# Attention, Fourier and MLP kernel on one core: xs·at behind ak·va on TensorE, y behind m2's copy on VectorE, xs2 without its wait for y

## The reference

```python
B, H, S, D = 4, 8, 768, 40
for t in range(S):
    y[:, :, t] = einsum('bhd,bhde->bhe', rt, state)
    Sa = einsum('bhde,bhe->bhd', state, at)
    state_decay = state * wt[:, :, None, :] - einsum('bhd,bhe->bhde', Sa, bt)
    state = state_decay + einsum('bhd,bhe->bhde', vt, kt)
# then: x = y as (B, S, 320); u = x + real(fft(fft(x, axis=1), axis=2));
# x = u + relu(norm(u) @ w_ch1) @ w_ch2; then a token MLP and a channel MLP
```

## The kernel before

| block | row in the profile | what it is | who reads it |
|---|---|---|---|
| m2 | ps<-mt,nn | step of the inverse | DVE mt<-ps,mt (L432) |
| rhs_v | pr<-va,ak | ak times va, 16 products of 64x40, fp32 | rhs_a adds to the same bank |
| n8 | ps<-nn,nt | last squaring, bf16 | DVE nn<-ps,eye (L436), "n8's copy" |
| rhs_a | pr<-xs,at | at times xs, added to rhs_v's bank | ACT rhs_b (L341) |
| ut | ps<-ident_a,u (L711) | 4 transposes of u | ACT ut (L356) |
| tokk | ps<-ident_a,kt (L719) | 4 transposes of kt | ACT tok_of |
| m3 | pp<-mt,nn | last product of the inverse | ACT minv (L335) |
| abk | pp<-at,bt and pp<-at,kt | first block of the next window | DVE aa, ak |

## Time and profile before

### The profile page before, as it was taken

How to read it: one execution, slowest core, us unless ns; L and a number is a source line. 1 busy time by engine, 2 the same in 40 slices (tenths; PEclk the granted TensorE clock), 3 DMA queues, 4 the chain that set the end, 5 groups by cost and what they waited for, 6 DMA issues and landing times. The chain is left out here.

```text
span 1011.8 us, 48583 instructions
## 1 busy us (share of the span) xinstructions
PE 958.3 (95%) x21467; PEld 911.6 (90%) x21468; DVE 500.4 (49%) x941; ACT 349.0 (34%) x758; POOL 301.7 (30%) x361
## 2 busy tenths in 40 slices
PE   6899999999999679998999999999999999999995
PEld 4788988888888568888999999999999999999995
DVE  4366677766767356765444333346733223322330
ACT  3466666665665433332221111232322112211220
POOL 6456655565566417705200000027500000000000
PEclk9999999999999999999999999999999999999998
DMA  7256666676665344302000000003100000000000
GB/s 250 101 185 210 196 198 202 196 229 209 199 211 174 96 122 156 102 1 68 25 0 0 0 0 0 0 0 107 37 1 20 20 0 19 19 19 6 13 19 19
DMA packets 50249, 86.80 MB, mean 86 GB/s; under 512 B 6066, under 2 KB 29746, under 8 KB 50194
## 3 DMA queue, kind: packets, MB, share of 16 engines
q1 hardware_dynamic: 48578, 81.96, 25.5%
q0 software_dynamic: 880, 3.69, 1.2%
q10 hardware_dynamic: 736, 0.48, 0.2%
HBM read 70.37 MB, written 7.86 MB: 77 GB/s over the span
## 5 line engine op out<-in xcount | busy, mean ns | idle before, releaser
L1412 ACT ACTIVATE d_h_hi<-d_bank 128x384 fp32r<-128x384 f32 x96 | 47.1, 491 | 200.1 <-PE d_bank L1494 200.1
L1449 DVE SCALAR_TENSOR_TENSOR d_h_lo<-d_bank,d_h_hi 128x384 fp32r<-128x384 f32 x96 | 53.5, 558 | 78.1 <-ACT d_h_hi L1412 78.1
L1508 PE MATMUL d_bank<-w_lo,d_h_hi 128*128 128x320 f32 x288 | 89.0, 309 | 0.0
L1508 PE MATMUL d_bank<-w_hi,d_h_lo 128*128 128x320 f32 x288 | 89.0, 309 | 0.0
L1508 PE MATMUL d_bank<-w_hi,d_h_hi 128*128 128x320 f32 x288 | 89.0, 309 | 0.0
L1412 ACT ACTIVATE c_h_hi<-c_bank 128x384 fp32r<-128x384 f32 x80 | 37.5, 489 | 146.4 <-PE c_bank L1494 146.4
L1508 PE MATMUL c_bank<-w_hi,c_h_hi 128*128 128x320 f32 x240 | 74.8, 312 | 0.0
L1508 PE MATMUL c_bank<-w_hi,c_h_lo 128*128 128x320 f32 x240 | 74.1, 309 | 0.0
L1508 PE MATMUL c_bank<-w_lo,c_h_hi 128*128 128x320 f32 x240 | 74.1, 309 | 0.0
L1461 DVE TENSOR_TENSOR d_o<-d_bank,u_all 128x320 f32<-128x320 f32 x24 | 11.8, 492 | 111.0 <-PE d_bank L1508 111.0
L1449 DVE SCALAR_TENSOR_TENSOR c_h_lo<-c_bank,c_h_hi 128x384 fp32r<-128x384 f32 x80 | 42.3, 554 | 40.9 <-ACT c_h_hi L1412 40.9
(11 more groups left out here) (265 smaller groups left out, 2792.1 us busy)
## 6 DMA issues: line engine op xcount, KB each, us to landing
e_raw<-in_e SPq DMA_DIRECT2D x72, 256.0 KB, 4.3
r_raw<-in_c SPq DMA_DIRECT2D x24, 768.0 KB, 4.3
tok<-tok_of SPq DMA_DIRECT2D x24, 320.0 KB, 2.7
e_raw<-in_e SPq DMA_DIRECT2D x24, 260.5 KB, 4.1
va<-in_c SPq DMA_DIRECT2D x24, 160.0 KB, 2.5
vb<-in_c SPq DMA_DIRECT2D x24, 160.0 KB, 2.7
attention_out<-yout SPq DMA_DIRECT2D x92, 40.0 KB, 2.0
stage<-in_moe_w_ch POOLq DMA_DIRECT2D x4, 640.0 KB, 6.9
```

The costliest lines, as they stand in the source:

```text
L1412: nc.scalar.activation(h_hi[:, m, :], bank[m % 4][:, 0:TW], ACT.Relu).then_inc(h_hi_done, 1)
L1449: nc.vector.scalar_tensor_tensor(h_lo[:, m, :], bank[m % 4][:, 0:TW], 0.0, h_hi[:, m, :].bitcast(F32), ALU.max, ALU.subtract).then_inc(h_l ...
L1508: last = nc.tensor.matmul(bank[4 + t % 2][:, 0:E], lhs, rhs, start=(m == 0 and i == 0), stop=(m == NM - 1 and i == 2))
```

## The change

Three things change, all in the tables. In ORDER_PE, rhs_a stands directly behind rhs_v and n8 behind it. In ORDER_DVE, y stands behind m2 (m2's copy) instead of ahead of it. In PORT_AFTER, the entry of xs2 is gone. No instruction is added or removed, and the code of the blocks stays the same but for its place in the file.

```diff
-ORDER_DVE = [... ("u", -3), ("xs", -2), ("y", -4), ("m2", -2), ("n8", -2), ("suff", 0), ("aa", -1),
+ORDER_DVE = [... ("u", -3), ("xs", -2), ("m2", -2), ("y", -4), ("n8", -2), ("suff", 0), ("aa", -1),
...
-            ... ("xsd", -2), ("m2", -1), ("rhs_v", -1), ("n8", -1),
-            ("rhs_a", -1), ("ut", -2), ("tokk", 0), ("m3", -1)]
+            ... ("xsd", -2), ("m2", -1), ("rhs_v", -1), ("rhs_a", -1),
+            ("n8", -1), ("ut", -2), ("tokk", 0), ("m3", -1)]
...
-PORT_AFTER = {"kt": ("suff", 0), "mt0": ("decay", 1), "xs2": ("y", -2)}
+PORT_AFTER = {"kt": ("suff", 0), "mt0": ("decay", 1)}
```

More of the change, by code:

```diff
@@ L30 @@
 ORDER_SP = [("store", -5), ("cp", -4), ("vb", -4), ("va", -2), ("e", 0), ("rr", -3)]
-ORDER_DVE = [("du2", -3), ("m1", -2), ("xt", -4), ("u", -3), ("xs", -2), ("y", -4), ("m2", -2), ("n8", -2), ("suff", 0), ("aa", -1),
+ORDER_DVE = [("du2", -3), ("m1", -2), ("xt", -4), ("u", -3), ("xs", -2), ("m2", -2), ("y", -4), ("n8", -2), ("suff", 0), ("aa", -1),
              ("ak", -1), ("rv", -3), ("decay", 0), ("ru", -3)]
@@ L35 @@
             ("res2", -2), ("y_s", -3), ("n2", -1), ("y_k", -3), ("sol2", -2), ("n2t", -1), ("y_b", -3), ("m1", -1), ("res3", -2),
[2 rows of a table removed]
+            ("n4", -1), ("upd_k", -3), ("upd_b", -3), ("n4t", -1), ("sol3", -2), ("xsd", -2), ("m2", -1), ("rhs_v", -1), ("rhs_a", -1),
+            ("n8", -1), ("ut", -2), ("tokk", 0), ("m3", -1)]
 ORDER_ACT = [("rhs", -1), ("m3", -1), ("ut", -2), ("du0", -1), ("tokd", 0), ("tokb", 0), ("res1", -1), ("tokk", 0), ("du1", -1),
@@ L690, in unit @@
                 last.then_inc(ready["rhs_v"], 1)
[L691 to L697, removed]
             if name == "rhs_a":
@@ L705, in unit @@
                 last.then_inc(filled["rhs_a"], 1)
+            if name == "n8":
+                take(n, "xsd", -1)
+                for j, par in halves:
+                    q = tok_half(par)
+                    last = mm(out[q, j * C:j * C + C], nt[2][q, j, :], nn[2][q, j, :])
+                    took(n, 2 * j + par, last, ("xsd", -1))
+                last.then_inc(filled["n8"], 1)
             if name == "ut":
```

## The result

| | before | after |
|---|---|---|
| median | 1015.12 us (4 runs, 1013.65 to 1015.89) | 1030.87 us (4 runs, 1028.68 to 1033.6) |
| ratio | | 1.0158, 95% interval 1.0129 to 1.0187 |
| the profiled execution, its time / span | 1013.78 / 1011.8 us | 1028.68 / 1026.7 us |

The changed kernel is slower, as forecast. The forecast was 1028.9 us with a range up to 1031.0; the median of these runs is 1030.87 us, and the ratio on the base of the prediction, 1015.53 us, gives 1031.6 us, so the loss was 16.0 us (13.1 to 19.0) where 13.4 us had been worked out. The two profiled executions are 14.9 us apart.

The account below looks back on a forecast made before the run. TensorE's in-order list was taken to bound the attention; 12.2 us from tokk's waits, 0.6 us in the second window and 0.58 us behind the loop gave 13.4 us on the 1015.53 us median: 1028.9 us, range 1020.5 to 1031 us.

Parts of the forecast that it names:

- rhs_a waits for rhs_v's end (313.48 and not 313.11): On TensorE, rhs_a would start no earlier after the swap, so n8 leaves a free place for one paid for.
- tokk 0.58 us later, through n8's copy: At the window's end, n8 shifts 0.86 us, less 0.28 us its copy had waited; tokk loads at 315.27, not 314.69.
- The whole of it reaches abk: tokk's full 0.58 us delays abk's products through m3; the 0.50 us from m3 to abk is TensorE's own step.
- Part 2: y behind m2's copy on VectorE: costs nothing, worth only the 0.28 us already taken off tokk's delay.
- the 0.28 us taken off: Time n8's copy had waited on VectorE for m2's copy, subtracted from n8's shift of 0.86 us.
- Part 3: xs2 without its wait on GpSimd: earlier start buys nothing; xs ends at 313.10 instead of 312.98, covered.
- The cover I named, rhs_a's 0.27 us: Slack left between xs's end at 313.10 on VectorE and rhs_a's need of it at 313.37.
- The smaller and the larger loss: Rivals: rhs_a starts at 313.11 or at sets abk (17%); xs late for rhs_a, 1031 to 1033 us (6%).
- The sum, 13.4 us: Total attention loss: tokk's wait 21 times at 0.58 us (12.2 us), second window 0.6, window behind the loop 0.58.
- the first window's term: Loop's first window: loss 0, at most 0.6 us, since TensorE stands 1.54 us inside ut while n8's copy ends.
- the 0.5 us for the median: Allowance for the median within the forecast's own range of 1026.5 to 1030.5 us.
- The case 'faster', 3.7 us: Rival: n8's copy stops being late on VectorE and tokk's 0.16 us wait goes, 23 times; 1011.8 us, 5%.

Follow-up runs that it names:

- n8_twice: The changed kernel with n8's 16 products run once more between rhs_v and rhs_a; window 13.82 us, median 1030.63 us, ratio 1.0159.
- own_bank: The changed kernel with n8's products in another PSUM bank, so m3 and not tokk waits for n8's copy; window 13.32 us, median 1016.14 us.
- swap_only: The kernel before with only TensorE's order changed, rhs_a ahead of n8; window 13.80 us, median 1025.45 us, ratio 1.0111.
- no_swap: The kernel before with y behind m2's copy and xs2 without its wait, TensorE's order kept; window 13.39 us, median 1019.89 us, ratio 1.0058.
- y_early: The kernel before with y ahead of xt on VectorE and xs2 without its wait; window 13.20 us, median 1012.30 us, ratio 0.9972.

## Why the prediction was right or wrong

**rhs_a waits for rhs_v's end (313.48 and not 313.11): right**, shown by n8_twice and by the idle time of 0.27 us. The prediction called the 0.11 us of the earlier trace rows "again" the same step as the 0.15 us of the earlier trace rows; inside the loop it is 0.15 us in the changed kernel too (312.71 to 312.86).

**tokk 0.58 us later, through n8's copy: right.** It is 0.59 us by the two timelines, and own_bank takes 0.47 us out of the window when tokk does not wait.

**The whole of it reaches abk: right.** abk moved by 0.58 us, the window from 13.22 to 13.79 us.

**Part 2 costs nothing: right. That it is worth the 0.28 us taken off: wrong.** swap_only leaves y ahead of m2's copy and has the same window (13.80 against 13.79 us), with VectorE idle for 0.49 us ahead of n8's copy. n8 comes so late through the swap that its copy is clear of m2's copy wherever y stands. The 0.28 us belong to the swap, and the sum stays the same.

**Part 3, xs2's start buys nothing and is covered: right, with a wrong size.** xs got longer by 0.18 us, not 0.12, since it starts 0.42 us into xs2 and still ends 0.35 us behind it. For this reason m2's copy came only 0.22 us earlier against rhs_v, where 0.3 to 0.4 us were forecast. The Trainium skill, "SBUF — State Buffer", "Who interferes with whom", calls the shared port pair an exclusive lock over which such a pair of instructions contends; its words "for the whole instruction" stand there for the 2-port modes. Taken for the whole of xs, as the prediction took them, xs would have ended 0.49 us behind xs2; the rows show 0.34 or 0.35 us in each kernel, so what is excluded is less than the instruction. The cover I named, rhs_a's 0.27 us, was not the only place to look: n8's copy, the third instruction behind xs on VectorE, had no cover at all in the old order, as no_swap shows.

**The smaller and the larger loss:** neither came by its mechanism. Measured on the median the time lies where the larger loss was priced (1031 to 1033 us), but xs was never late for rhs_a. In the equal windows the granted clock stayed at 1.00 (77.53 to 312.02 us); low clock stood in the loop's first window (0.54 from 34 to 41 us in the first profile of the changed kernel, 1.00 in that of the kernel before) and behind the loop.

**The sum, 13.4 us: right for the equal windows, and close for the attention in part by luck.** The last y moved by 13.7 us on the mean of three profiles each. In the first profiles rhs_v number 2, 3 and 23 starts its products at 48.10, 61.53 and 325.85 us before, and at 49.91, 63.73 and 339.61 us after; the last y starts at 369.11 and 383.67 us. By stretches, the loss is:

| stretch | forecast, us | the profiled pair, us | mean of three, us |
|---|---|---|---|
| to the second rhs_v (the loop's first window) | 0, at most 0.6 | 1.8 | 0.6 |
| to the third rhs_v | 0.6 | 0.4 | 0.4 |
| the next 20 windows | 11.6 | 11.6 | 11.6 |
| from the 23rd rhs_v to the last y | 1.2 | 0.8 | 1.1 |
| together | 13.4 | 14.6 | 13.7 |
| from the last y to the end | 0 | 0.3 | -0.4 |

**The step that failed is what stands outside the equal windows: the first window's term, put at 0 (at most 0.6 us), and the 0.5 us for the median.** In the profiled pair the first term measured 1.8 us, with the clock as just said; in the three pairs of profiles it is 1.8, 0.8 and -0.8 us. The second term was too small: the profiled pair is 14.9 us apart and the medians 15.75 us, and the ratio on the base of the prediction makes it 16.0 us. The changed kernel's profiled execution (1028.68 us) was the fastest of its four, and the others, of which there is no trace, took 1029.84, 1031.89 and 1033.6 us at mean granted clocks of 0.984, 0.980 and 0.977, against 0.985. Where their time went is not known.

Twelve runs of the kernel before went from 1010.72 to 1018.6 us in one series, and the medians of the changed kernel in two series were 1030.87 and 1025.83 us. The first ratio, 1.0158, says 16.0 us and the second, 1.0135, says 13.7 us; the intervals overlap, and 13.4 us lies in both. So it is in part chance that the time came out above the range and not in it. With 2 to 3 us for the spread, and not 0.5, the upper end would have been at 1032.4 to 1033.4 us instead of 1031.0. The forecast's own range is also added up wrongly: 22 to 24 windows by 0.54 to 0.62 us and 0.5 us either way give 1026.9 to 1030.9 us, not 1026.5 to 1030.5.

**The case 'faster', 3.7 us: wrong in its price.** In y_early tokk's wait went, as this case wanted, and the window gained 0.02 us.

**Open:** why y_early and swap_only come out 1.5 to 2.5 us below what their windows say, and no_swap and n8_twice as much above. The difference stands mostly behind the loop, in windows that are written out. From the start of the 23rd rhs_v to the last y it is 42.3 to 43.3 us in the kernel before and 43.2 to 44.5 us in the changed one, but 42.4 us in swap_only, 41.1 and 39.7 us in y_early, 45.1 and 46.2 us in no_swap and 46.9 us in n8_twice. The granted clock falls there in every profile; from 330 to 390 us it is 0.94 to 0.97 before, 0.91 in all three profiles of the changed kernel and 0.89 both in the first y_early, which is short, and in no_swap, which is long. So the clock alone does not order them, and no run took the stretch apart.

## What to carry to other kernels

A block between two others that depend on each other may be running in a wait that no list of waits shows; look for a next block that starts a fixed time after the end of the one before, and not right behind its loads. Before a short chain (products, copy, next reader) is moved towards its reader, add its latency and see what is left to cover it. And when a wait goes away, look for the second wait that ends within hundredths of a microsecond of it: here it took 0.14 of the 0.16 us. Last, a sum over equal windows says nothing of the first one and of those behind the loop: give them a range of their own, from more than one profile.

## What the runs showed of the hardware

- TensorE that waits for its own products loads again 0.15 us after the last of them ends (312.05 + 0.66 = 312.71, loads at 312.86), with 0.27 us of idle time in the loads (the changed kernel; swap_only shows 0.16 us).
- A VectorE operation on two SBUF inputs that started 0.42 us into a GpSimd operation of 0.74 us took 0.67 instead of 0.49 us, and ended 0.35 us behind it (the changed kernel); in the second window of the loop, where it started 0.58 us in, it took 0.51 us and ended 0.35 us behind it too.
- The low clock at the start of the program (0.50 for some 7 or 14 us) fell at different places in executions of the same kernel; with it inside the loop's first window, that window of the changed kernel took 16.26 and 16.12 us, with most of it ahead of the window 14.60 us.
